# Row maxima subtracted on GpSimd, and one exponential a unit on ScalarE, in an attention and dense kernel on one core

## The reference

```
k_sum = max of k over blocks of 32 tokens;  v_sum = mean of v over the same blocks   (24 blocks)
scores_l = q k^T / 8, kept only where |i - j| < 16, else -1e9
scores_s = q k_sum^T / 8 + log(32)
a = softmax(concat(scores_l, scores_s))                  # row maximum subtracted, sum + 1e-9
x = a @ concat(v, v_sum)                                 # heads side by side: (2, 768, 512)
u = x + (x^T U V)^T ;  y = u + relu(u @ w_ch1) @ w_ch2   # 512 -> 2048 -> 512
y_prev = y shifted by one token
k2 = relu((mu_k*y + (1-mu_k)*y_prev) @ w_k) ; out = sigmoid((mu_r*y + (1-mu_r)*y_prev) @ w_r) * (k2*k2 @ w_v)
```

## Time and profile before

| | |
|---|---|
| time of 3 runs, median | 533.92 us (531.57 to 534.18) |
| time of the profiled execution | 534.35 us |
| span of the profiled execution | 532.6 us |
| busy, PE / DVE / ACT / POOL | 505.1 / 259.7 / 202.1 / 26.4 us |
| mean granted TensorE clock | 0.99 |
| mean of POOL's 7 copies of key windows (L315) | 1147 ns |
| first matmul of the dense groups starts at | 66.16 us |

### The profile page before, as it was taken

How to read it: one execution, slowest core, us unless ns; L and a number is a source line. 1 busy time by engine, 2 the same in 40 slices (tenths; PEclk the granted TensorE clock), 3 DMA queues, 4 the chain that set the end, 5 groups by cost and what they waited for, 6 DMA issues and landing times.

```text
span 532.6 us, 8482 instructions
## 1 busy us (share of the span) xinstructions
PE 505.1 (95%) x3392; PEld 468.5 (88%) x3392; DVE 259.7 (49%) x621; ACT 202.1 (38%) x401; POOL 26.4 (5%) x47
## 2 busy tenths in 40 slices
PE   3379799999999999999999999999999999999997
PEld 2356799999999999999999999999989989988985
DVE  3378445545545435536355363586653552562501
ACT  4256354234333324323142231555562561561410
POOL 3065000010000000000000000000000000000000
PEclk9998799999999999999999999999999999999999
DMA  8987614311202202213224132310001001001001
GB/s 287 298 217 222 197 41 142 125 23 70 90 1 81 81 1 80 78 42 119 79 90 146 42 120 79 119 40 1 1 9 51 1 7 54 1 0 61 0 1 59
DMA packets 15272, 42.02 MB, mean 79 GB/s; under 512 B 1792, under 2 KB 4224, under 8 KB 15232
## 3 DMA queue, kind: packets, MB, share of 16 engines
q1 hardware_dynamic: 14944, 41.08, 24.1%
q10 hardware_dynamic: 288, 0.39, 0.2%
HBM read 37.13 MB, written 3.15 MB: 76 GB/s over the span
## 4 chain that ended last, share of the span: by engine, by line
PE 90%; DVE 4%; DMA 3%; issue 1%; ACT 1%; SPq 0%; DVEq 0%; ACTq 0%
PE ps L675 87%; PE ps L735 2%; DMA vwin<-vm 2%; DMA kT<-in_kT 1%; PE ps L678 1%; DVE P L514 1%; DVE u_lo L639 1%; ACT xa L455 1%; DVE xa L633 1%; DVE vsum L504 1%; DVE kmax L498 0%; PE ps L719 0%; ACT m_hi L435 0%; DVE u_lo L557 0%; DVE mixr L534 0%
## 5 line engine op out<-in xcount | busy, mean ns | idle before, releaser
L675 PE MATMUL ps<-u_hi,w_hi 128*128 128x384 f32 x256 | 87.3, 341 | 0.0
L675 PE MATMUL ps<-h_hi,w_hi 128*128 128x384 f32 x256 | 87.1, 340 | 0.0
L675 PE MATMUL ps<-u_hi,w_lo 128*128 128x384 f32 x256 | 85.9, 336 | 0.0
L675 PE MATMUL ps<-h_hi,w_lo 128*128 128x384 f32 x256 | 85.9, 336 | 0.0
L675 PE MATMUL ps<-u_lo,w_hi 128*128 128x384 f32 x256 | 85.9, 336 | 0.0
L675 PE MATMUL ps<-h_lo,w_hi 128*128 128x384 f32 x256 | 85.9, 335 | 0.0
L418 ACT ACTIVATE h_hi<-ps 128x384 fp32r<-128x384 f32 x64 | 31.4, 491 | 119.1 <-PE ps L675 119.0
L596 DVE SCALAR_TENSOR_TENSOR h_lo<-ps,h_hi 128x384 fp32r<-128x384 f32 x64 | 35.7, 557 | 70.5 <-ACT h_hi L418 70.3
L601 DVE TENSOR_TENSOR yT<-ps,yT 128x384 f32<-128x384 f32 x64 | 35.6, 556 | 54.0 <-PE ps L675 53.9
L675 PEld LDWEIGHTS ps<-u_hi,w_hi 128*128 128x128 f32 x256 | 48.1, 188 | 1.8 <-issue 1.2
L675 PEld LDWEIGHTS ps<-h_hi,w_hi 128*128 128x128 f32 x256 | 48.0, 188 | 1.5 <-issue 1.5
(11 more groups left out here) (84 smaller groups left out, 733.6 us busy)
## 6 DMA issues: line engine op xcount, KB each, us to landing
wraw<-in_w SPq DMA_DIRECT2D x42, 512.0 KB, 3.5
vwin<-in_vw SPq DMA_DIRECT2D x8, 580.5 KB, 6.4
kT<-in_kT SPq DMA_DIRECT2D x8, 400.0 KB, 6.5
vT<-in_vT SPq DMA_DIRECT2D x8, 384.0 KB, 4.8
out<-scratch SPq DMA_DIRECT2D x12, 256.0 KB, 2.0
qt<-in_qT SPq DMA_DIRECT2D x7, 384.0 KB, 6.7
vwin<-vm SPq DMA_DIRECT2D x8, 145.1 KB
U<-in_U SPq DMA_DIRECT2D x1, 384.0 KB, 10.3
```

The costliest lines, as they stand in the source:

```text
L675: return nc.tensor.matmul(o, lhsT, rhs, start=start, stop=stop)
```

## The change

GpSimd subtracts the row maxima from a whole unit in one operation over 4 x 120 columns, once all four maxima are there (`less_max`), ahead of ScalarE, which then makes one exponential of the 480 columns without a bias. TensorE's transposes wait for that one. GpSimd's other work is put in a new order around the 24 subtractions, `split_V`, `split_part` and `ones` among it.

```diff
--- before.py
+++ after.py
@@ -115,6 +115,7 @@
         k_in, q_in, v_in, bc_in = [[sem(f"{n}_in{i}") for i in range(NBUF)] for n in ("k", "q", "v", "bc")]
         q0_in, small_in, mu_ok = sem("q0_in"), sem("small_in"), sem("mu_ok")
         kmax_done, ksum0_done, ksum_done, vm_done = sem("kmax_done"), sem("ksum0_done"), sem("ksum_done"), sem("vm_done")
+        less_done = sem("less_done")
         vt_in, vsum_done = [sem("vt_in0"), sem("vt_in1")], sem("vsum_done")
         kw0_done, kw_done, vs_step, vs_ok, mhi_done = sem("kw0_done"), sem("kw_done"), sem("vs_step"), sem("vs_ok"), sem("mhi_done")
         s_done, m_done, e_done, t_done, pt_done, pv_done = (sem("s_done"), sem("m_done"), sem("e_done"), sem("t_done"),
@@ -337,23 +338,58 @@
                 nc.gpsimd.tensor_tensor(w_slot(w_lo, j), wraw[:, j, :], w_slot(w_hi, j).bitcast(f32), ALU.subtract)\
                     .then_inc(wlo_done, 1)
 
-            ones(0)
+            def less_max(v):
+                pool.wait_ge(m_done, 4 * v + 4)
+                p, m = P[v % 3][:, :, :], nmax[v % 3][:, :]
+                nc.gpsimd.tensor_tensor(p, p, bass.AP(m.tensor, m.offset, [list(m.ap[0]), list(m.ap[1]), [0, COLS]]), ALU.subtract)\
+                    .then_inc(less_done, 1)
+
+            less_max(0)
             windows(1)
             summaries(1)
+            ones(0)
+            less_max(1)
             ones(1)
+            less_max(2)
             windows(2)
+            less_max(3)
             summaries(2)
+            less_max(4)
             ones(2)
+            split_V()
+            less_max(5)
+            windows(3)
+            less_max(6)
+            summaries(3)
+            less_max(7)
             split_part(0)
-            windows(3)
-            split_V()
-            summaries(3)
+            less_max(8)
+            ones(3)
+            less_max(9)
+            windows(4)
             split_part(1)
-            ones(3)
-            for p in range(4, 2 * PAIRS):
-                windows(p)
-                summaries(p)
-                ones(p)
+            less_max(10)
+            summaries(4)
+            ones(4)
+            less_max(11)
+            windows(5)
+            summaries(5)
+            ones(5)
+            for v in range(NU, NU + 3):
+                less_max(v)
+            windows(6)
+            for v in range(NU + 3, NU + 5):
+                less_max(v)
+            summaries(6)
+            ones(6)
+            less_max(NU + 5)
+            windows(7)
+            for v in range(NU + 6, NU + 8):
+                less_max(v)
+            summaries(7)
+            ones(7)
+            for v in range(NU + 8, 2 * NU):
+                less_max(v)
 
         @block.scalar
         def _(act):
@@ -361,10 +397,9 @@
             act.dma_start(qt[0][:, 4 * HALF:S], qT[0, :, 4 * HALF:S]).then_inc(q_in[0], 16)
 
             def exps(v):
-                for k in range(4):
-                    act.wait_ge(m_done, 4 * v + k + 1)
-                    p = P[v % 3][:, k, :]
-                    nc.scalar.activation(p, p, ACT.Exp, bias=nmax[v % 3][:, k:k + 1], scale=-1.0).then_inc(e_done, 1)
+                act.wait_ge(less_done, v + 1)
+                p = P[v % 3][:, :, :]
+                nc.scalar.activation(p, p, ACT.Exp, scale=-1.0).then_inc(e_done, 1)
 
             def copy_PT(v):
                 act.wait_ge(t_done, v + 1)
@@ -731,7 +766,7 @@
             def transpose_p(v):
                 need(pe, pt_done, v)
                 for k in range(4):
-                    pe.wait_ge(e_done, 4 * v + k + 1)
+                    pe.wait_ge(e_done, v + 1)
                     last = nc.tensor.transpose(ps[0:COLS, 512 * PB + 128 * k:512 * PB + 128 * k + 128], P[v % 3][:, k, :], ident[:, :])
                 last.then_inc(t_done, 1)
```

## The result

The changed kernel takes 540.3 us (539.93 to 540.87 in 4 runs), beside 532.75 us of the kernel before in the runs that go with it: ratio 1.015, 95% interval 1.01 to 1.02. It is slower by 7.55 us. The profiled execution took 540.35 us with a span of 538.6; that of before took 534.35 with 532.6.

A forecast was written before the change was run, and what follows sets the result against it. Batch 0's attention was taken as latency-bound, TensorE as full from 66 us. Batch 0's 7.9, the clock's 1.0 and batch 1's 0.8 sum to 9.7 us on 534.35, less 0.43: 543.6 us, range 539 to 548.5.

The forecast's parts named there:

- as summed: Whole kernel: the summed terms hold, 543.6 us, between 540.5 and 546.5; chance 0.63.
- less is lost: Rival: units catch up or POOL's splits find slack, a third to two thirds of 9.7 us, 537.1 to 540.4; chance 0.12.
- What bounds it: Batch 0's attention goes by latency, so added loop time from 21.5 to 66 us counts whole; afterwards only TensorE stalls count.
- Before 21.5 us: Start of the kernel: early subtractions hidden behind the transfer ending at 21.4 us; cost nothing.
- Unit 4 and unit 5: Batch 0: subtractions queued behind summaries(2) and split_V make the product of unit 4 start at 39.6, 5.7 us late.
- Units 6 and 7: Batch 0, product 4 to product 6: set by TensorE and DVE at 7.7 us, nothing more lost at the same clock.
- The two splits: Batch 0, units 8 to 10: subtractions queued behind split_part(0) and split_part(1), 2.15 us more after 1.5 absorbed.
- Batch 1: Batch 1: subtraction fits ACT's wait except where L615 holds POOL; TensorE waits 0.4 us twice, 0.8 us in sum.
- The clock: Batch 0 after product 4: idle TensorE may bring the low clock level, nothing to 2.3 us, taken as 1.0.
- the low clock throughout: Rival: low clock holds nearly the whole stage between 33 and 65 us, 5.4 instead of 1.0 us, 548; chance 0.18.

The follow-up runs named there:

- batch0_new: Changed kernel with subtraction and single exponential only in batch 0's 12 units, batch 1 as in the kernel before: ratio 1.0166 to the kernel before, median 540.83 us.
- batch1_new: The change only in batch 1's 12 units, batch 0 and POOL's order there as in the kernel before: ratio 1.0007 to the kernel before.
- order_only: Changed kernel's POOL order without the subtractions, the four exponentials with a bias kept: ratio 1.0001 to the kernel before.
- all_aside: Changed kernel with split_V, split_part(0), split_part(1) and summaries(2) moved so that no batch 0 subtraction queues behind long POOL work: ratio 1.0025 to the kernel before.
- late_reductions_aside: all_aside with the same move of DVE's reductions as in late_reductions: ratio 0.9998 to the kernel before, median 531.74 us.
- rounded_output: Changed kernel with the subtraction writing fp32r in place of f32: one execution of 541.38 us.
- late_reductions: Kernel before with DVE's u_low of iteration 9 ahead and block_sum(5), block_max(5) moved to iteration 11: ratio 0.9961 to the kernel before, median 530.24 us.
- two_full_operands: Changed kernel with tile P itself as the subtraction's second operand instead of the repeated row maxima: one execution of 540.6 us.
- all_aside_longer: all_aside with POOL copying P onto itself ahead of the subtraction in units 1 to 11: ratio 1.0049 to the kernel before.

## Why the prediction was right, point by point

The range 539 to 548.5 holds 540.3, and sign and mechanism hold: most of the loss is the queue on POOL in batch 0. The size is less good than that. The loss was 7.55 us by the medians and 6.0 between the profiles, where the sum had 9.7. The case that I gave 0.63, "as summed", began at 540.5, so 540.3 lies just under it, and by number alone in the case "less is lost" (537.1 to 540.4), to which I gave 0.12. Only the width of the range hides that. Between the profiles, the 3.7 us too many are 1.4 of units 4 and 5, 1.25 of the splits, 0.55 of the clock and 0.45 of batch 1. Some of it is luck of the clock, as said at each. Term by term:

**What bounds it.** Right. batch0_new and batch1_new put the loss where the prediction did, and order_only shows that the queue harms only through what stands in it. ACT's 15 us won nothing on balance, in batch 0 too: all_aside and late_reductions_aside have them and are slower than their counterparts without. The relief without the serial step was not run.

**Before 21.5 us: nothing.** Nearly: all the added work was hidden, but the first product started at 22.09, 0.56 late. It still waited for the transfer (issued at 12.36, not 12.14, and 0.35 us longer), and in order_only and batch1_new it began at 21.63 and 21.68. In the other kernels that subtract in batch 0 it was 21.8 to 22.4 and once 23.3 (rounded_output), in late_reductions, which doesn't, 21.94; so how much of it belongs to the change is open.

**Unit 4 and unit 5: 5.7 us.** Measured 4.3 (38.20 against 33.88). The step is right and two terms of it are off. The subtraction took 0.99 us, not 1.17. And block_max(2) ended at about 30.0, not 30.71, since TensorE's clock rose earlier: the second product took 0.69 us at 25.33, where before it took 1.14 at 24.86. That is luck: in batch0_new, whose program up to there is the same, and in two_full_operands, whose subtractions are as long, the second product took 1.13 us, and the product of unit 4 began at 39.43 and 39.14, close to my 39.6 and 5.6 and 5.3 late.

**Units 6 and 7: nothing beside the clock.** Product 4 to product 6 took 9.15 us, not 7.7, so 1.45 of low clock, between my 0 and 2.3. The windows show it, with the granted clock third from the right, and so does the product with U, which took 1.60 us before:

```profile
28.00:41.50 13.50, 7.53 (x116) 5.85 (x117) 7.09 (x34) 4.04 (x8) 9.16 (x10) 0.90 0.87 215
```

```profile
41.29 2.05 PE L710 MATMUL ps<-xnat,U 128*128 128x128 f32 x12
```

**The two splits: 2.15 us.** From product 6 to product 9 it took 12.37 us instead of 10.01, so 2.4 more, where I had 3.6; before had run part of this at the low clock, and after did not. From product 9 to the turns it took 2.3 instead of 3.8: 1.5 absorbed, as forecast. From the turns to the dense work it took 9.77 instead of 10.81, another 1.0 of clock that before had lost. Together 4.3 + 1.45 + 2.4 - 1.5 - 1.0 = 5.65 us, the whole delay of the first dense matmul, at 71.81 where I had about 75.

**Batch 1: 0.8 us.** Measured 0.35 from the first dense matmul to the end, and between -0.2% and 0.3% by batch1_new. All three subtractions beside L615 were held, the one at group 4 too, which I had let go first.

**The clock: 1.0 us.** Between the profiles it was 1.45 after unit 4 less the 1.0 that before had lost at its end, so 0.45. This is the term that the sum could not size, because the kernel before has such a loss of its own. In the 29 runs of the last comparison, those of before with a mean granted clock of 0.999 or 1.000 took 529.9 to 532.2 us, those with 0.994 or less 533.8 to 535.6; the other eight, with 0.996 or 0.997, lie between at 531.2 to 532.8. The profiled execution, with 0.99, was one of those with 0.994 or less, and I summed from it. All four runs of the changed kernel had 0.987 to 0.990, and all six of batch0_new 0.984 to 0.990: with these waits the low level came back in every run. More waiting alone does not force it: of the 12 runs of all_aside_longer six had 1.000. So profile to profile the change costs 6.0 us, and median to median 7.55. Of the rivals, that of the low clock throughout did not come about: 50 to 60 us was at 0.97.

## What to carry to other kernels

Before moving work to an idle in-order engine, list what it will be queued behind, and price that queue: here twelve operations of 0.99 us in the latency-bound stage cost 7.5 us, and moving the engine's long operations into its own idle time took it down to 1.3 with the same subtractions. Relief of an engine that waits for its input won nothing here. Before summing from a profile, see which clock it had: two executions of one kernel differ here by up to 5.7 us (529.9 to 535.6), nearly as much as the change costs. In a stage that goes by latency, a wait that is removed shows the next one right behind it, so the list of waits has to be followed until one of the moved things lies in real idle time.

## What the runs showed of the hardware

POOL was held though its record begins first. At group 4 of the changed kernel the rows are

```profile
86.60 2.10 POOL L344 TENSOR_TENSOR P<-P,nmax 128x480 f32<-128x480 f32 x1 [9.46 <-DVE nmax L549]
86.64 1.20 DVE L650 TENSOR_TENSOR w_lo<-wraw,w_hi 128x1024 fp32r<-128x1024 f32 x1
```

The `L650` of this kernel is the L615 of before. DVE's operation kept its usual 1.2 us and POOL's took 1.1 us more than elsewhere. SBUF, State Buffer, of the Trainium skill (Who interferes with whom) has the one that issues first keep the port; a start in a record within 0.04 us of the other's did not say which that is. Whether DVE issued first here, or POOL did and lost all the same, the rows do not show. In the other two held cases DVE's record begins first, by 0.16 us in each.

The same code does not always get the same clock. Up to 41 us batch0_new and the changed kernel have the same program, and their products of units 3 and 4 started at 33.81 and 39.43 in the one and 32.56 and 38.20 in the other. The later one ran the second product at 1.13 us where the other ran it at 0.69 (rows of batch0_new):

```profile
25.43 1.13 PE L705 MATMUL ps<-vwin,PT 120*64 120x65 f32 x16
...
33.81 0.69 PE L705 MATMUL ps<-vwin,PT 120*64 120x65 f32 x16 [2.48 <-ACT PT L402]
...
39.43 1.13 PE L705 MATMUL ps<-vwin,PT 120*64 120x65 f32 x16 [2.44 <-ACT PT L402]
```
